# Seventy TensorE products with unread results in the routing, and VectorE's gates and low places moved to the end of the last slot

## The reference

```python
# attention: complex decaying state per head, B=4, H=8, S=768, D=48
S_re, S_im = ar * S_re - ai * S_im + k v^T, ar * S_im + ai * S_re
y[t] = q[t] @ S_re
# dense network, 3072 tokens, 384 -> 2048 -> 384
h = x @ w_in;  x2 = (h * tanh(softplus(h))) @ w_out
# experts, E=8, 384 -> 1024 -> 384
logits = x2 @ w_gate + modality_bias[modality_id]
e = argmax(logits);  gate = softmax(logits)[e]
out[tokens of e] = gate * (relu(x2[tokens of e] @ w1[e]) @ w2[e])
```

## Time and profile before

| | |
|---|---|
| median of 3 runs | 1034.48 us (1034.05 to 1034.8) |
| the profiled execution | 1036.13 us, of which the span is 1034.4 us |
| TensorE busy with products | 968.0 us, 94% of the span |
| VectorE busy | 712.5 us, 69% |
| ScalarE busy | 574.0 us, 55% |
| GpSimd busy | 90.0 us, 9% |
| mean granted clock | 0.97 |

### The profile page before, as it was taken

One profiled execution on the slowest core, in us unless ns is written; L12 is line 12 of the kernel. 1 busy time (PEld: TensorE's weight loads), 2 busy tenths in 40 slices (PEclk: granted clock), 3 DMA queues, 4 the chain that ended last, 5 costly groups with the idle time before them and its releaser, 6 DMA issues. The chain is left out here.

```text
span 1034.4 us, 18775 instructions
## 1 busy us (share of the span) xinstructions
PE 968.0 (94%) x6528; PEld 936.7 (91%) x6529; DVE 712.5 (69%) x1301; ACT 574.0 (55%) x1069; POOL 90.0 (9%) x149
## 2 busy tenths in 40 slices
PE   5889899999999999999999999987499999999996
PEld 3778798999999999999999999987399999999996
DVE  4666998988888988888888968875443333653432
ACT  6556887876776876777776665453022223222221
POOL 2000000000000000000000000000022222442221
PEclk9899999999999999999999999999589999999999
DMA  9702211221221221122121010000341111431110
GB/s 205 217 8 33 39 39 24 50 52 39 40 62 39 39 62 40 39 62 40 39 63 39 10 46 1 1 23 26 130 153 38 46 38 38 163 141 38 38 46 23
DMA packets 146227, 58.65 MB, mean 57 GB/s; under 512 B 131321, under 2 KB 140551, under 8 KB 146160
## 3 DMA queue, kind: packets, MB, share of 16 engines
q1 hardware_dynamic: 139056, 42.61, 17.1%
q0 software_dynamic: 3904, 10.44, 3.2%
q10 hardware_dynamic: 3200, 4.72, 1.2%
HBM read 48.21 MB, written 10.03 MB: 56 GB/s over the span
## 5 line engine op out<-in xcount | busy, mean ns | idle before, releaser
L1856 PE MATMUL bank<-xg_t,w_sb 128*128 128x128 f32 x1296 | 151.1, 277 | 1.4 <-DVE xg_t L1449 1.4
L1856 PEld LDWEIGHTS bank<-xg_t,w_sb 128*128 128x128 f32 x1296 | 150.5, 194 | 1.8 <-issue 1.8
L1630 PE MATMUL bank<-x_hi,w_in_hi 128*128 128x384 f32 x384 | 141.9, 369 | 4.9 <-ACT hid L762 3.0
L1649 PE MATMUL bank<-w_out_hi,g_hi 128*128 128x392 f32 x384 | 141.1, 367 | 0.0
L1630 PE MATMUL bank<-x_hi,w_in_lo 128*128 128x384 f32 x384 | 131.6, 343 | 0.0
L1630 PE MATMUL bank<-x_lo,w_in_hi 128*128 128x384 f32 x384 | 131.3, 342 | 0.0
L1649 PE MATMUL bank<-w_out_hi,g_lo 128*128 128x392 f32 x384 | 130.6, 340 | 0.0
L1649 PE MATMUL bank<-w_out_lo,g_hi 128*128 128x392 f32 x384 | 130.6, 340 | 0.0
L945 ACT ACTIVATE he<-bank 128x128 f32<-128x128 f32 x216 | 60.0, 278 | 110.9 <-PE bank L1856 106.7
L762 ACT ACTIVATE hid<-bank 128x384 f32<-128x384 f32 x128 | 62.3, 487 | 82.0 <-PE bank L1630 81.7
L949 ACT ACTIVATE o_sb<-bank,gate_now 128x384 f32<-128x384 f32 x27 | 15.7, 581 | 117.8 <-PE bank L1867 117.8
(11 more groups left out here) (286 smaller groups left out, 2094.4 us busy)
## 6 DMA issues: line engine op xcount, KB each, us to landing
w_sb<-in_moe_w_dram SPq DMA_DIRECT2D x8, 1536.0 KB, 6.5
ab<-in_a_re_dram SPq DMA_DIRECT2D x24, 192.0 KB, 2.9
ab<-in_a_im_dram SPq DMA_DIRECT2D x24, 192.0 KB, 3.2
x_rows<-x_sb ACTq DMA_DIRECT2D x8, 576.0 KB, 3.0
qk_raw<-in_q_dram SPq DMA_DIRECT2D x22, 192.0 KB, 3.3
qk_raw<-in_k_dram SPq DMA_DIRECT2D x22, 192.0 KB, 3.3
v_in<-in_v_dram SPq DMA_DIRECT2D x22, 192.0 KB, 2.8
w_out_sb<-in_moe_w_out_dram SPq DMA_DIRECT2D x4, 768.0 KB, 6.7
```

Of the source, the lines that this page charges most:

```text
L1630: last = mm(bank_h[f % 2][:, 0:TT], w[:, kk, f * P:(f + 1) * P], x[:, m % 2, kk], start=(kk == 0 and i == 0), stop=(kk == KD - 1 and i == 2))
L1649: last = mm(bank_x2[t][:, 0:DE], g[:, u % RING, f % QF, t * P:(t + 1) * P], w[:, f], start=(f == 0 and i == 0), stop=(f == FT - 1 and i == 2))
L1856: last = mm(bank_h[f % 2][:, 0:P], w1_sb[par][:, kk, f * P:(f + 1) * P], xg_t[:, kk], start=(kk == 0), stop=(kk == KD - 1))
```

## The change

- `stay_awake(count)` is new: `count` products of 128x128 float32 (identity by `earlier`) into the bank `bank_h[0]`, whose content nobody reads any more. It is called four times: 16 before the wait for the last choice (`chosen_ready`), 25 after the rank products, 7 after the order products, 22 before the first `turn_tokens`. Each product is a pair of a weight load and a multiplication in two records, as those of L1856 are.
- On VectorE `place_ranks` of the 18 groups moves from gap 4 to gap 22 of the last slot. `gates` and `low_places` of the 18 groups leave the slot and stand after the last `times`, before VectorE's wait for the copied results; `low_places` is one instruction for all 18 groups there.

```diff
-    RANK_AT, GATE_AT, LO_AT = 4, 6, (8, 10)
+    RANK_AT = 22
@@ VectorE, slot(m)
                     if m == NT - 1 and g == RANK_AT:
                         dve.wait_ge(ranks_ready, 1)
                         place_ranks(straight, bank_a, 0, GE)
-                    if m == NT - 1 and g == GATE_AT:
-                        dve.wait_ge(exped, 1)
-                        gates(straight, 0, GE)
-                    if m == NT - 1 and g in LO_AT:
-                        dve.wait_ge(y_ready, NCH)
-                        n = LO_AT.index(g)
-                        low_places(straight, GE // 2 * n, GE // 2 * (n + 1))
@@ VectorE, after the slots
             times(NT * NQ - 1)
+            dve.wait_ge(exped, 1)
+            gates(straight, 0, GE)
+            dve.wait_ge(y_ready, NCH)
+            low_places(straight, 0, GE)
             dve.wait_ge(slow_known, 1)
@@ TensorE, after the slots
+            def stay_awake(count):
+
+                for _ in range(count):
+                    mm(bank_h[0][:, 0:P], ident[:], earlier[:], start=True, stop=True)
+
+            pe.wait_ge(h_copied[0], FT // 2 * NT)
+            stay_awake(16)
             pe.wait_ge(chosen_ready, 2)
...
+            stay_awake(25)
             for g in range(NG):
...
             last.then_inc(order_ready, 1)
-
+            stay_awake(7)
             pe.wait_ge(order_done, 1)
...
+            stay_awake(22)
             turn_tokens(0)
```

## The result

| | before | after |
|---|---|---|
| median | 1034.51 us (1034.05 to 1034.8, 4 runs) | 1026.16 us (1025.24 to 1027.86, 4 runs) |
| ratio to before | 1 | 0.9907, 95% interval 0.9881 to 0.9933 |
| profiled execution, its span | 1036.13, 1034.4 | 1025.24, 1023.5 |
| mean granted clock | 0.968 | 0.986 |

The changed kernel is 8.35 us faster by the medians. The predicted 1026.4 is 0.2 us from it and the range holds it. The part in the slot came as forecast; in the routing the mechanism is another than the one forecast, as the rows show.

What follows compares the result with a forecast made beforehand. TensorE was taken as busy nine tenths of the time, with only gaps and slow clock to win. Tokens 6.1 us earlier plus 2.0 for a warm first layer gave 8.1 off 1034.48, so 1026.4 us, range 1024.6 to 1029.9.

Steps and rivals of the forecast that it cites:

- Part 1: Last slot: moving 5.35 us off VectorE's list removes TensorE's 3.01 us wait and its slow products, 4.65 us gained.
- The cover: VectorE's pauses take the moved work: `weigh` at most 0.5 us late; 3.5 us at the end fit a 7.01 us pause.
- The rank products: L1823 to L1825 in the routing find the clock high after 16 products: 1.55 us becomes about 0.85, 0.7 less.
- list of waits: TensorE's waits: 9.2 us for gathered tokens, 4.9 for the sums, 3.0 for ScalarE's `take` in the last slot.
- The order products: L1830 in the routing: clock falls early, 1.5 us done warm and 7.7 at half rate, 9.2 us instead of 10.52.
- The gather's landing: Gather issued 3.85 us after w1's load, landing interpolated as 10.7 us after it, at 743.85, 6.1 us earlier.
- The first layer warm: L1856 of the first tile takes 5.36 us instead of 7.66; 2.0 us counted, bounds 0 and 2.3.
- The sum: 6.1 us from earlier tokens plus 2.0 from the first layer: 8.1 us at L1867 of the first tile, kept afterwards.
- rival C: Gather gets ahead and w2 sets the second layer's start: 1024.7 us, or 1026.3 if the clock falls again; chance 0.15.
- Rival B: Clock lost twice in the routing: L1830 takes 10.5 us, tokens late, L1856 not kept warm; only 5.35 left, 1029.1; chance 0.26.
- Rival D: The slot's wait stays because ScalarE's list caused it: 4.65 us less gain, 1031.1; chance 0.07.
- Rival E: Extra products run at half clock and delay the routing: 4.8 us slower, 1039.3; chance 0.04.

Runs made afterwards that it cites:

- list_only: The changed kernel without any of the 70 extra products, only VectorE's list moved: 1031.23 us, ratio 0.9956 to before.
- rank_at_4: The changed kernel with `place_ranks` back at gap 4, only `gates` and `low_places` out of the slot: 1026.23 us, ratio 0.9919 to before.
- narrow_41: The changed kernel with the first 16 and next 25 products 66 columns wide instead of 128: 1031.72 us, ratio 0.9956 to before.
- products_only: The changed kernel with VectorE's list put back as before, only the 70 products added: 1032.94 us, ratio 0.9971 to before.
- late_45: The changed kernel with 45 instead of 25 products before the order products: 1027.12 us, ratio 0.9907 to before.
- cover_38: The changed kernel with 38 instead of 22 products before the tokens are turned: 1027.57 us, ratio 0.9923 to before.
- no_25: The changed kernel without the 25 products between rank and order products: 1027.45 us, ratio 0.9926 to before.

## Why the prediction came out right, and where it did not

**Part 1, 4.65 us: right.** Measured 4.6 by list_only, and 4.65 between the two first traces. The cover held as costed: `weigh` behind `place_ranks` started 0.42 us later than it could have, and the pause at the end took in `gates` and `low_places` with 3.79 us left. Of the 5.35 us moved, 3.6 are enough (rank_at_4).

**The rank products, 0.7 us: right in size.** 0.76 for 1.55. Unforeseen was the 1.31 us of issue before the first 16 products (the chain of after), where the prediction had them follow without idle time. The room just held both: the ranks started at 716.63, VectorE's choice was there at 716.56. The prediction's list of waits also left out the 7.0 us of L1830 for `carried`, which it uses as room further on.

**The order products, "it falls early, 9.2 us": wrong.** They took 5.57, warm whole, in nine traces. The step argued from the earlier trace rows, where 10.5 us of such products do not bring a low clock back, to the belief that they do not hold a high one behind 1.4 us of idle time. That products cannot raise the clock does not say how long they may run before it falls: narrow_41 shows 1.6 us, products_only 1.2, and the nine others at least 5.5, all nine behind 25 or more wider products, but so was products_only. The idle 1.4 us do not decide it either: seven of the nine have them. What decides between the one case and the nine stays open.

**The gather's landing, by interpolation, at 743.85: wrong by 3.25 us.** It follows from the step before, for the gather went out 0.46 us after w1's load and not 3.85. The interpolation itself was fair: for offsets of 0.5, 3.1, 4.2 and 5.2 us behind w1's issue the landings were 7.3 to 9.3, 9.8, 11.8 and 11.4 to 11.6 us after it (10.3 was read from such points for 3.1, in late_45's expectation). The DMA rows for 738:739 of the changed kernel (packets, MB, share of the 16 engines) show both queues moving at once:

```profile
q1 hardware_dynamic: 62, 0.25, 59.8%
q0 software_dynamic: 48, 0.13, 35.4%
```

The gather's packets move where w1's load ends (q1 ran at 98 to 100% in the two microseconds from 735) and w2's begins. The Trainium skill (DMA: Bandwidth & Descriptors, Queues, rings and completion order) says that the engines take turns between queues, packet by packet. This slice agrees with turns being taken. But the gather took 7.4 us beside the weights for 3.9 alone, and in the kernel before it moved no packet for 4 us while q1 ran full, so the rule alone does not tell when it lands; by what the late gather is held up, no run shows.

**The first layer warm, worth 2.0 us: wrong twice in this kernel.** It was cold, 8.08 us, because with warm order products the 29 products end at 736.9, 3.7 us before the tokens. The prediction had worked out 742.7 for their end, from a clock that was low. And where it was warm beside early tokens, it was worth nothing (cover_38): w2's landing and the split come after it. The bound "0 to 2.3" held the truth at its lower end. With tokens as late as the prediction had them the term would have been near 1.3 to 1.6 (no_25 against list_only and before), so there it was too large by half a microsecond only. The choice of 2.0 looked at `he_lo` of before, which ended 1.6 us before L1867, and did not ask when the same VectorE would have done w2's split if all but w2 came earlier. The prediction asked that in rival C alone.

**The sum: right by two errors that cancel.** Forecast 8.1 us at the second layer, measured 8.4 in the trace (9.0 less the 0.62 of chance) and 8.35 in the medians. The tokens came 3.3 us sooner than forecast, the first layer took 2.7 us longer. That these two meet is luck. That the total fell so near is a little more than luck: from w1's issue on, w2 and its split set a lower bound for the second layer, 17.3 to 18.6 us in the traces with early tokens, which a warm first layer could not have gone below. w1's issue came at 732.73, forecast 733.15. What happened is rival C in its first half, to which the prediction gave 0.15: L1830 warm whole and "ends with the run table" (730.1 and 730.5), the gather 0.46 us after w1's load (0.7 forecast), w2 there at 745.29 (744.4), the second layer at 751.34 (750.5). C's fall of the clock in the second layer did not come, which took 4.38 us; the clock fell before the first layer instead. Cover_38 is C whole, with 2.4 us of waiting and a second layer of 5.99. So the 1026.3 that C gives with its fall is met by another fall than C's.

**Rival B** (0.26, 1029.1) needs cold order products and a cold first layer. No_25 has only the first and gives 1027.45. The trace of products_only has both, and its 43.7 us from the slot are no less than the 43.2 of before: with the list moved as well, that leaves the 4.65 us of the slot, for the 5.35 that B has. So nothing here says that B's price was too high. **Rival D** fell with list_only. **Rival E** can be had, by narrow products: narrow_41, 1031.7.

**Still open:** why the clock held through the order in nine traces and fell in one, and how much of the scatter between 1025.0 and 1027.9 of the changed kernel comes from executions in which it fell. Only one execution of each kernel was traced. No run leaves out the first 16 or the last 29 products by themselves. That the 29 win nothing in the changed kernel is argued from its cold first layer; behind a late gather they did keep the clock (no_25).

## What to carry to other kernels

Before crediting a change with time won in front of a wait for several things, work out for each of them when it would come if all others came at once; here w1's issue plus w2's landing plus its split gave 17.3 to 18.6 us, and a warm first layer did not go below it, while splitting the load and its conversion in two won 3.3 us more. Products that only keep TensorE's clock should be as wide as the ones that were seen to raise it in the same kernel; here narrow ones, busy in every row, stood at a clock of 0.50 and then in the way. And a wait that one engine has for a second can come from the list of a third: 4.6 us of this change come from small instructions moved into a pause of the engine that does them.

## What the hardware showed that was not expected

- TensorE can read 1.00 busy for 30 us at a granted clock of 0.50 (narrow_41, 717 to 747). The Trainium skill (TensorE: Matmul & The Clock Gate, Part 1: The HAM clock gate) says that the gate follows how busy the engine has been lately. In this trace the busy share of the rows did not foretell the clock: it read 1.00 through the 26 us of 66-column products at 0.50, and 1.00 through the 4.7 us of 128-column products after which the clock was 1.00 again (in products_only it was back 2.1 us after such products began, at 741.83).
- The gather of 128 rows lands in 3.9 us alone, in 6.9 to 8.8 us when issued some 0.46 us after w1's load (seven traces; 7.4 in that of after), and 6.2 to 7.6 us after its own issue when that load is 4 to 5 us old.
- TensorE has 0.9 to 1.4 us of issue between the last product of the slot and the first of the 16, and up to 1.7 before the first layer, in which it waits for nothing that the profile shows. Products set there to keep the clock do not reach into this time.
